# State change behind every block of 32 rows instead of gram blocks, from chunk 2 on, in a delta-rule attention followed by two feed-forward layers

## What is computed

```python
B, H, S, D = 4, 8, 768, 48
k_n = k / (norm(k) + 1e-06)
state = zeros((B, H, D, D))
for t in range(S):
    y[:, :, t] = einsum('bhd,bhde->bhe', q[:, :, t], state)
    v_old = einsum('bhde,bhd->bhe', state, k_n[:, :, t])
    state = state + beta_t * einsum('bhd,bhe->bhde', k_n[:, :, t], v[:, :, t] - v_old)
x = y as (3072, 384)
h = x @ w_in1                    # 384 x 2048
g = h where h >= 1, 0 where h <= -1, (h + 1)**2 / 4 between
x = g @ w_out1                   # 2048 x 384
r = maximum(x @ w_in2, 0);  result = (r * r) @ w_out2
```

## Time and profile before

| | us |
|---|---|
| median of 3 runs (lowest, highest) | 998.61 (996.92, 1001.49) |
| the profiled execution | 998.77 |
| its span | 997.0 |
| PE busy | 980.3 |
| DVE busy | 583.1 |
| ACT busy | 412.1 |
| layer 1 beside attention, tile 2 (first product to first product) | 254.17 to 349.94 |

### The profile page before, as it was taken

The page is one execution under the profiler, slowest core; times in us unless marked ns, Lnnn a source line. Parts: engine busy times, 40 slices in busy tenths (PEclk is TensorE's granted clock), DMA queues, the critical chain, the costliest instruction groups (busy, mean ns, idle before and its releaser), DMA issues.

```text
span 997.0 us, 24738 instructions
## 1 busy us (share of the span) xinstructions
PE 980.3 (98%) x10486; PEld 805.1 (81%) x10486; DVE 583.1 (58%) x1461; ACT 412.1 (41%) x717; POOL 38.2 (4%) x53
## 2 busy tenths in 40 slices
PE   6999999999999999999999999999999999999998
PEld 6777788788888888888888888888888888888887
DVE  7879778777777687769535773433434334334332
ACT  5667434433444434434345553333333233333332
POOL 5700000000000000000000000000000000000000
PEclk8899899999999999999999999999999999999999
DMA  6522132003200410020003411001010010000000
GB/s 218 191 86 65 58 94 77 9 19 94 76 15 18 116 49 18 19 65 33 3 12 128 158 63 64 1 1 64 1 64 1 1 63 1 30 3 1 32 1 32
DMA packets 28413, 50.96 MB, mean 51 GB/s; under 512 B 2320, under 2 KB 15760, under 8 KB 28304
## 3 DMA queue, kind: packets, MB, share of 16 engines
q1 hardware_dynamic: 28304, 49.39, 15.4%
HBM read 39.94 MB, written 9.44 MB: 50 GB/s over the span
## 4 chain that ended last, share of the span: by engine, by line
PE 94%; DVE 2%; ACT 2%; issue 1%; DMA 0%; ACTq 0%; DVEq 0%
PE psum L1179 39%; PE psum L1155 38%; PE psum L949 3%; PE psum L924 2%; PE psum L1026 2%; PE psum L966 2%; PE psum L975 1%; PE psum L1071 1%; PE psum L902 1%; PE psum L1063 1%; PE psum L1058 1%; PE psum L1099 1%; PE psum L1079 1%; DVE act_g L1448 1%; DVE tmp L1320 0%
## 5 line engine op out<-in xcount | busy, mean ns | idle before, releaser
L1179 PE MATMUL psum<-g_hi,w 128*128 128x512 f32 x1152 | 393.4, 397 | 0.0
L1155 PE MATMUL psum<-x_hi,w 128*128 128x512 f32 x1152 | 386.4, 390 | 0.0
L1454 DVE TENSOR_TENSOR g_lo<-act_g,g_hi 128x512 fp32r<-128x512 f32 x192 | 132.5, 690 | 218.1 <-ACT g_hi L789 218.0
L1179 PEld LDWEIGHTS psum<-g_hi,w 128*128 128x128 f32 x1152 | 216.9, 188 | 51.0 <-issue 2.2
L1155 PEld LDWEIGHTS psum<-x_hi,w 128*128 128x128 f32 x1152 | 216.2, 188 | 45.6
L789 ACT ACTIVATE g_hi<-act_g 128x512 fp32r<-128x512 f32 x192 | 121.4, 632 | 279.3 <-PE psum L1179 242.9
L1179 PE MATMUL psum<-g_lo,w 128*128 128x512 f32 x576 | 225.3, 391 | 0.0
L1155 PE MATMUL psum<-x_lo,w 128*128 128x512 f32 x576 | 224.1, 389 | 0.0
L1448 DVE TENSOR_TENSOR act_g<-act_g 128x512 f32<-128x512 f32 x96 | 66.4, 692 | 112.9 <-ACT act_g L782 112.9
L1155 PEld LDWEIGHTS psum<-x_lo,w 128*128 128x128 f32 x576 | 108.1, 188 | 22.2
L1179 PEld LDWEIGHTS psum<-g_lo,w 128*128 128x128 f32 x576 | 108.6, 189 | 20.8
(11 more groups left out here) (113 smaller groups left out, 628.6 us busy)
## 6 DMA issues: line engine op xcount, KB each, us to landing
kt_sb<-in_k_t SPq DMA_DIRECT2D x24, 256.0 KB, 4.2
qt_sb<-in_q_t SPq DMA_DIRECT2D x24, 256.0 KB, 3.4
ring<-in_v_s SPq DMA_DIRECT2D x24, 192.0 KB, 2.6
kn_sb<-in_k_n SPq DMA_DIRECT2D x18, 256.0 KB, 4.1
between_layers<-y_out SPq DMA_DIRECT2D x6, 768.0 KB, 3.6
x_sb<-between_layers SPq DMA_DIRECT2D x6, 768.0 KB, 5.6
result<-y_out SPq DMA_DIRECT2D x5, 768.0 KB, 3.9
wi_st<-in_w_in SPq DMA_DIRECT2D x7, 384.0 KB, 3.6
```

The source lines that it names most:

```text
L1155: ins = pe.matmul(h_ps[n % 2][:, :], w_in_part(layer, f // GW, part)[:, kt, fs], x[:, kt, :], start=(kt == 0 and j == 0), stop=(kt == KT - ...
L1179: ins = pe.matmul(acc[kt][:, :], w_out_part(layer, f // GW, part)[:, f % GW, ds], g[n % 2][:, :], start=(f == 0 and j == 0), stop=(f == NF ...
L1454: dve.tensor_tensor(g_lo[n % 2][:, :], act_g[n % 2][:, :], g_hi[n % 2][:, :].bitcast(F32), ALU.subtract).then_inc(g_lo_ready, 1)
```

## The change

From chunk 2 on (`BY_BLOCK = 2`) the states are brought up to date behind every row block, so that the residual of the next block needs only the current state. Two sets of states exist: the outputs of a chunk still read the states at its start. Chunks 0 and 1 are as before. The second set, a ring of keys by rows (`ks_sb`, four buffers, loaded from a new input `k_s`) lie where the gram blocks were; a copy of u in row layout (`u_rows`) lies in a buffer of `kn_sb`.

```diff
+BY_BLOCK = 2
...
-            at = {9: 0, 10: 1, 11: 2, 14: 3} if t == 0 else {7: 0, 8: 1, 9: 2, 14: 3}
+            at = {9: 0, 10: 1, 11: 2, 14: 3} if t == 0 else {2: 0, 4: 1, 5: 2, 14: 3}
...
-        def gram_at(t, f):
...
+        def blocks_of(n):
+
+            return 0 if n < BY_BLOCK else NB if n < NC - 1 else NB - 1
...
-            return m if m is not None and m < ITEMS - B else None
+            return m if m is not None and m < BY_BLOCK * B else None
...
+            def load_ks(k):
...
+                    sp.wait_ge(change_done, 2 * B * (changes_to(*divmod(k, NB)) - RING + 1))
+                sp.dma_start(ks_sb[k % RING].rearrange("p h e -> p (h e)"), k_s[k]).then_inc(ks_loaded[k % RING], 16)
...
+            def solved_rows(k):
+
+                act.wait_ge(t_done, B * (k + 1 - NB))
+                wait(act, change_done, 2 * B * changes_to(*divmod(k, NB)))
...
+                act.activation(u_rows, ts_ps(k)[:, 0:DM].rearrange("p (h e) -> p h e", e=D), ACT.Copy).then_inc(u_rows_ready, 1)
...
                 square_part(n)
+                if changed_at(t, f) is not None:
+                    solved_rows(changed_at(t, f))
                 k = solve_at(t, f)
                 if k is not None:
                     for b in range(B):
                         solved(k, b)
...
+            def change_by_rows(k, turn):
+
+                n, i = divmod(k, NB)
+                pe.wait_ge(u_rows_ready, changes_to(n, i) + 1)
+                pe.wait_ge(ks_loaded[k % RING], 16 * (n - BY_BLOCK + 1))
...
+                for a in range(HP):
+                    for hp in range(2):
+                        for b in (turn, turn + 2):
+                            rows = block_rows(b)
+                            at = (turn * HP + a) * D
+                            ins = pe.matmul(change_ps(b)[hp * DP:hp * DP + D, at:at + D], ks_sb[k % RING][rows, 2 * a + hp, :],
+                                            u_rows[rows, 2 * a + hp, :], start=True, stop=True)
...
-                k = residual_at(t, f)
-                if k is not None and t:
-                    substitute(k)
...
+                    if kt == 0 and n < STEPS and f and changed_at(t, f - 1) is not None:
+                        change_by_rows(changed_at(t, f - 1), 1)
...
-                if t == 0 and residual_at(t, f) is not None:
+                if residual_at(t, f) is not None:
                     substitute(residual_at(t, f))
+                if changed_at(t, f) is not None:
+                    change_by_rows(changed_at(t, f), 0)
...
+            def running_states(k):
+
+                n, i = divmod(k, NB)
+                dve.wait_ge(change_done, 2 * B * (changes_to(n, i) + 1))
...
+                for hp in range(2):
...
+                    change = psum[part, 6:8, 0:2 * HP * D].rearrange("p c (a e) -> p c a e", e=D)
+                    dve.tensor_tensor(of_two(state_of(n, 1)), of_two(state_of(n, i)), change, ALU.add).then_inc(running_ready, 1)
...
-                k = residual_at(t, f)
-                if k is not None and t:
-                    residual(k)
...
-                if k is not None and not t:
+                k = residual_at(t, f)
+                if k is not None:
                     residual(k)
+                k = changed_at(t, f)
+                if k is not None:
+                    running_states(k)
```

More of the change, by code:

```diff
@@ L117, in delta_rule_then_two_moe @@
         ring = sa("ring", [P, RING, H, D])
-        gram = [sa(f"gram{b}", [P, H, LATE]) for b in range(B)]
+        gram_or_states = sa("gram_or_states", [P, B, H, LATE])
         kq = [sa(f"kq{i}", [P, 2, HP, P]) for i in range(QUERIES)]
@@ L175, in staged, with state_of @@
             return w_i[:, :, :], w_o[:, :, :]
+        gram = [gram_or_states[:, b, :, :] for b in range(B)]
+        behind_gram = gram_or_states[:, :, :, :].rearrange("p b h t -> p (b h t)")
+        other_s = behind_gram[:, 0:PAIRS * 2 * D].rearrange("p (a h e) -> p a h e", h=2, e=D)
+        ks_sb = [behind_gram[:, PAIRS * 2 * D + i * DM:PAIRS * 2 * D + (i + 1) * DM].rearrange("p (h e) -> p h e", e=D)
+                 for i in range(RING)]
+        u_rows = kn_sb[:, 0, :, :].rearrange("p h e -> p (h e)")[:, 0:DM].rearrange("p (h e) -> p h e", e=D)
         def gram_at_chunk(n):
             return gram1 if n == 1 else gram
+        def state_of(n, i):
+            first, other = (s_bd[:, :, :, :], other_s) if n % 2 == 0 else (other_s, s_bd[:, :, :, :])
+            if n < BY_BLOCK:
+                return s_bd[:, :, :, :]
+            return first if i == 0 else other
         def kq_of(m, hp):
@@ L260, in delta_rule_then_two_moe @@
         state_ready = sem("state_ready")
+        other_zero = sem("other_zero")
+        ks_loaded = [sem(f"ks_loaded{i}") for i in range(RING)]
+        u_rows_ready = sem("u_rows_ready")
+        change_done = sem("change_done")
+        running_ready = sem("running_ready")
         x_ready = sem("x_ready")
@@ L638, in _ @@
             low_parts(3)
+            pool.wait_ge(first_s_done, HALVES * (NB - 1))
+            pool.memset(other_s, 0.0).then_inc(other_zero, 1)
             for n in range(1, NC - 1):
@@ L811, in first_step @@
                         solved(k, b)
-                if t == 0 and gram_at(t, f) is not None:
-                    gram_out(gram_at(t, f))
                 if f == NF - 1 and t + 1 < NTT:
@@ L819, in first_step @@
                     g_high(n)
-                    if t and gram_at(t, f) is not None:
-                        gram_out(gram_at(t, f))
                     beside(t, f)
@@ L1025, in solve @@
                         rows = block_rows(b)
-                        ins = pe.matmul(t_ps[rows, j * D:(j + 1) * D], xc[rows, place(i, j), :],
+                        ins = pe.matmul(ts_ps(k)[rows, j * D:(j + 1) * D], xc[rows, place(i, j), :],
                                         ring[rows, k % RING, j, :], start=True, stop=True)
```

129 lines of the change are left out of this document (80 added, 49 removed).

## The result

The changed kernel took 1001.33 us in the median of 20 runs (lowest 998.19), the kernel before 999.39 in 20 runs. The profiled execution took 1001.78 us, its span is 1000.1. One run of each kernel, 3145.38 and 1085.72 us, stands far above its others and moves neither median.

What follows compares the result with a forecast made beforehand. PE's queue was taken as the bound: 998.8 us profiled, plus 3.6 for PE's own work and 1.2 for its waits, gave 1003.6 us, about 0.5% slower. The range was 993 to 1012.

Steps and rivals of the forecast that it cites:

- What bounds the kernel: Whole kernel: PE's queue is the bound, busy 980.3 of 997.0 us; PE does not wait in tile 2.
- insertions: Pieces put between PE's wide matmuls: each costs 0.24 us beside its own matmuls; tiles 1 to 4 go from 51 to 92.
- The price of a turn: PE, half a block's state change, 16 matmuls in 32 passes: 24 ns a pass, 0.77 us; 30 turns with insertions 30.3 us.
- PE's own sum: PE's added, split and removed work: 30.3 + 2.8 - 29.5 = +3.6 us, with bounds -7.2 and +12.6.
- rival 2: Cheap turns and a chain from solve to solve shorter than reckoned, so no waits: -7.2 us alone, 991.6; chance 0.14.
- The ring: Two-step chain from solve over ACT and DVE to next solve, 12.8 or 12.0 us; PE waits 1.2 us in tiles 1-3.
- PE's pair of steps: PE's work per two steps: four wide groups, solve, substitution and two turns with insertions, 12.3 us.
- Rival 1: A pass costs 12.7 ns, but the solve-to-solve chain holds PE up 6.0 us in three tiles: 997.6, no change; chance 0.20.
- Rivals 3 and 4: Third: a turn costs 1.07 us, 1011.4, chance 0.16. Fourth: `running_states` 1 us later, about +9, 1012, chance 0.08.
- turns near 0.4: then look whether the solves of steps 8, 10 and 12 wait for the residual: Sign in PE's timeline that the forecast is wrong: waiting solves mean the first rival, none the second.
- Hidden work: Loads, ACT's copies, masks and POOL's memset cost nothing; DVE's extra load is otherwise hidden, with 414 us without work.

Runs made afterwards that it cites:

- r_early: Changed kernel with DVE's residual moved ahead of the second inverse piece and low part from tile 1 on; 995.79 us, ratio 0.9964.
- p_again: Changed kernel with the 64-wide block products of the program's start done once more in step 1 of tile 4; 1000.49 us, one run.
- w_rows: Changed kernel with each turn's matmuls reordered, all eight of one batch, then all eight of the other; 1004.66 us, ratio 1.0053.
- r_long: Changed kernel with one unused 128x512 DVE operation added ahead of each running_states; 1008.36 us, ratio 1.0093.
- m_turns: r_early with both turns of a state change put behind the second product; 997.7 us, ratio 0.9987.
- m_turns_late: Changed kernel with both turns of a state change behind the second product, residual left behind the low part; 1001.51 us, ratio 1.0022.
- w_64: Changed kernel with the stationary side of a turn's matmuls 64 columns wide instead of 48, except the last head; 1002.66 us, ratio 1.0035.
- m_both: m_turns with the substitution of a chunk's first block moved behind the keys by queries of step 5; 996.83 us, ratio 0.9977.
- best: r_early with the substitution of a chunk's first block moved behind the keys by queries of step 5; 994.67 us, ratio 0.9941.
- r_copies: r_early plus the added DVE operation, with ACT's four copies of u behind its high part in steps 6, 8, 10, 12; 996.59 us, ratio 0.9982.

## Why the prediction was wrong

**What bounds the kernel** was right: PE's queue. Tiles 1 to 4 have 51 insertions before and 92 after, as counted, and the sizes of the insertions (0.24 us, some 0.2 inside a first product), of the removed pieces and of the moved ones were right. In r_early, where PE does not wait in tiles 1 to 4 beyond 0.3 us at step 2, tile 2 is 94.7 us. The same sum with the measured turn: 65.4 for the 32 groups of wide matmuls, 21.0 for the pieces that stay, each with the 0.09 us ahead of it, 8 turns of 0.51 + 0.09 = 4.8, and 24 insertions with 0.15 behind each = 3.6, together 94.8. With the 0.3 at step 2 it is 0.4 us too high.

**The price of a turn** is the first mis-sized term. I took 0.77 us by the row, measured is 0.51. Over 30 turns that is 7.8 us, and PE's own sum becomes -4.2 in place of +3.6. The step that failed was the choice between bounds: I preferred the row that was most alike in its places of the array and did not ask whether it ran unhindered. It stood at the start of the program, where PE ran at the lower level of its clock (p_again, above) and stopped for keys, and I divided the row's length, not the distance between starts, as the rows are meant to be read. The same shape at the full level costs 19.7 ns a pass, and three quarters of that would have been 14.8, against 15.9 measured. My reason for the choice, that two and four places cost the same, set 33.4 ns of the earlier trace rows, at the full level, beside those 32 ns at the lower one. At one level it is 33.4 against 19.7. The page "TensorEngine Tiling (Array Packing)" (Tiling Modes, Key Properties) of the Trainium skill, named beside rival 2, says that different tiles work in parallel. The trace agrees as far as it goes: in w_rows neighbours in one row group, and in one bank, cost 41% more.

**The ring** was built rightly and its waits were mis-sized by the same error. It was said to be 12.8, then 12.0 and 12.0 us long; between the starts of the solves of tile 2 it measured 12.67, 12.12 and 12.10 (from 286.97 over 299.64 and 311.76 to 323.86). Against PE's pair of steps with a cheap turn, 11.7 us (measured in r_early, where nothing waits), that is 1.0 + 0.4 + 0.4 of waiting in each of tiles 1 to 3, where I had 0.4 by a pair of 12.3. With 0.44 in tile 4, which I had excluded, and the waits at step 2, which I had not seen, some 6.7 us of waits stand in place of 1.2. (The 11.5 us that I gave the ring of tile 4 are not the sum of its named terms either: 10.4 and 0.4 make 10.8.) That gives back most of what the cheap turns save. The two errors have opposite signs: -7.8 and +5.5. They leave 2.3 us less than forecast, +2.5 in place of +4.8, against 1.9 between the medians and 1.5 by the stages. The rest is in part the second turns' insertions (15 at some 0.04 less, an estimate). That the time still came near the forecast is luck: one error took most of the other back.

**The rivals.** Rival 1, cheap turns and a ring that closes up, is the case that happened, in price (0.51 for its 0.41) and in place. It had 2.0 us of waits a tile, 1.8 were measured. Its time, 997.6, was low because a turn is 0.10 us dearer than its bound (3.0 us) and because tile 4 waits too. Rival 2, cheap turns and no ring, is the case of r_early, where the residual begins 10.7 us behind the solve's start in place of 12.1. It took an edit to get it, and its gain is half of what the rival had: 3.5 us between the medians and not 7.2, again because of the turn's price. Rivals 3 and 4 did not come about. The reading that would tell them apart ("turns near 0.4: then look whether the solves of steps 8, 10 and 12 wait for the residual") was the right one.

**Hidden work** held: no wait for `ks_loaded`, none for the second states, the clock full in tiles 1 to 4. What I passed over was a product of step 2, now at a place where it waits for ACT's copy of the diagonal blocks (0.3 us a tile). "DVE has 414 us without work" was true and worth nothing: r_long shows that an operation in the ring costs its full length all the same.

## What to carry to other kernels

Where engines work through fixed orders, list the closed chains from one use of a result to the next, and compare their length with the bound engine's time for the same round. A saving on the bound engine is kept only down to the longest of them. In such a chain look for what stands ahead of a step and is not needed by it: moving one subtraction ahead of an unrelated one gave 5.8 us here, more than the whole change moved. And before a row is used as a price, see whether it ran with its inputs at hand and at which level of the clock. Where the profile has no record of the clock, the length of a pass whose time at both levels is known tells it, as 364 and 245 ns did here. A shape that is timed at the start of a program is no price for its middle.

## What the runs showed of the hardware

The same small fp32 matmuls cost 22.5 ns a pass in an order that uses two column halves of one row group and one bank in turn, and 15.9 in one that uses two row groups, two column halves and two banks; which of the two counts was not separated. Sixteen more stationary columns in 14 of 16 matmuls cost 2.5 ns a pass.

At the start of the program TensorE runs at its lower level though the profile prints 1.00 for the stretch: a 48x96 pass takes 364 ns up to 13.2 us and 245 from 13.5 us on in the kernel before, and 364 again where the lower level is on record.

A second group of matmuls into the same banks from other row groups, made to wait for the first, begins 0.32 us late (m_turns).

Tile 0 takes 95.1, 96.7 or 98.2 us for the same instructions. In the stretch from 98 to 150 us the mean granted clock is 1.00 in the executions of the first kind (w_rows, m_turns_late, p_again), 0.97 in those of the second (w_64, m_turns, m_both), 0.93 in those of the third (r_early, best, r_copies and others). The clock is the number behind the busy times of PE, PEld, DVE, ACT and POOL:

```profile
98.00:150.00 52.00, 49.98 (x944) 39.88 (x943) 42.89 (x118) 23.87 (x41) 0.95 (x1) 1.00 0.34 104
```

```profile
98.00:150.00 52.00, 50.00 (x934) 40.03 (x936) 39.50 (x100) 21.45 (x39) 0.95 (x1) 0.93 0.25 73
```

The first row is the changed kernel (clock 1.00, tile 0 in 95.1 us), the second the kernel before (0.93, 99.0 with its one gram block more). What PE did ahead of it is a wait of about 2 us at the first solve beside layer 1; behind that wait the clock falls to its lower level, 1.2 GHz, for a while in some executions and not in others. In the kernel before, the wait (2.00 us) ends at 101.42 and the clock falls at 102; in the changed kernel's profile it (2.02 us) ends at 106.00 and the clock stays full. Together with the stretch ahead of tile 0 (59.2 to 62.8 us for the same instructions) this is the scatter of the profiled times, and a comparison of single runs of these kernels is mostly a comparison of that.
